# Second MoE of a fused attention and MoE kernel: no row gather in the last unit, no split of weight chunks for an expert that does not exist

## The chip, the cores and the metric

The kernel runs on one core of one Trainium2 chip. The metric is the device time of one execution in microseconds, here the median of three runs. Times "at 422.2" are microseconds from the start of the profiled span.

## What is computed

Three stages follow one another: attention with a local window and global columns, a soft MoE (every slot sees every token), and a top-1 MoE. The change lies wholly in the third, which is this (cut):

```python
logits = x @ w_gate                      # x (3072, 512), 8 experts
expert_idx = np.argmax(logits, axis=1)
gate_w = softmax(logits)[arange(N), expert_idx]
for e in range(E):
    mask = expert_idx == e
    if not mask.any():
        continue
    h = np.maximum(x[mask] @ w1[e], 0.0)
    out[mask] = gate_w[mask, None] * (h @ w2[e])
```

Only the experts that got tokens are computed; how many these are is known at run time alone. The kernel calls that number `used`, and an expert's place in the order of work its `rank`.

## The kernel before, in words

The attention output is stage one's, and x, the input of the third stage, is a product of the 32-slot combine weights with slot outputs. The third stage therefore gathers rows of combine weights (`c_rows` in HBM, 128 floats for a token) and not rows of x. Tokens are sorted by expert into tiles of 128, two tiles are a unit, and the units of all ranks are numbered through (`u`).

One unit goes so. GpSimd gathers the unit's two tiles of rows into `Cg` with two indirect DMAs (`gather`, L1486, each with its index taken from `src1`, which a small copy at L1480 fills). TensorE transposes them (`turn`, L1546), ScalarE copies the transposed rows to `CgT` (L1716), TensorE multiplies them into the folded first weights (`hidden`, L1557), ScalarE takes the ReLU into `hh` (L1724), VectorE makes the low part `hl` (L1913), and TensorE multiplies with the expert's second weights, high and low part, three products for each of eight chunks of the hidden width (`tile`, L1626 to L1628). VectorE scales the tile by its gate (L1986), and GpSimd stores it with an indirect DMA to the token's row of the output (L1513, index in `dst1`, filled at L1509). The work is pipelined by one unit: while TensorE does the products of unit u it also does `turn(u + 1)` and `hidden(u + 1)`, and GpSimd issues the gather for unit u + 2 before the stores of unit u. After the last unit `hidden` still runs once, for a unit that is not there, on whatever was gathered.

The second weights of rank r lie in slot `r & 1` of `w2h` (high part) and `w2l` (low part). Those of ranks 0 and 1 are split in place. Those of rank r + 2 are loaded to `raw` and split in four chunks when rank r is done: ScalarE copies a chunk to `w2h` (L1788, in `rank_done`), VectorE subtracts it from `raw` into `w2l` (L2011). The number of chunks at the end of a rank comes from `chunks_at_end`: four if rank r + 2 exists, else one.

The order of the work is the order in which each engine's code is written, in loops over ranks and units whose bounds are loaded from SBUF at run time (`count`, L1395; `plan`, L1387; `all_units`, L1399). The engines meet by semaphores. At the end of the program every engine runs a DRAIN and then a barrier; the records of both stand under L129. Before that GpSimd waits until all stores have landed (`stored`), reads the number of units (L1399), and waits for all gathers.

Of the kernel before, what the change touches and what calls it, by code (L numbers as in the profile page):

```python
# [15 lines left out]
F32 = mybir.dt.float32  # L16
# [3 lines left out]
ALU = mybir.AluOpType  # L20
# [39 lines left out]
W2CH = 4  # L60
# [1163 lines left out]
def top1_moe(nc, ctx, sb, psum, sem, block, sp_passed, ident, ones, Rsel, wg_sb, mem, STR, CT, counting,  # L1224
# [23 lines left out]
    w2h = sb(st, "w2h", [P, 2, WSIZE], F32R)  # L1248
    w2l = sb(st, "w2l", [P, 2, WSIZE], F32R)
# [19 lines left out]
    act = sb(st, "act", [P, NE])  # L1269
# [34 lines left out]
    raw = mem[:, 0, :]  # L1304
# [38 lines left out]
    v2_loaded = [sem("v2_loaded_first"), sem("v2_loaded_second")]  # L1343
# [3 lines left out]
    w2_high = sem("w2_high")  # L1347
    w2_low = sem("w2_low")
    src_copied = sem("src_copied")
    dst_copied = sem("dst_copied")  # L1350
    gathered = sem("gathered")
# [5 lines left out]
    y_quarter = sem("y_quarter")  # L1357
# [6 lines left out]
    act_passed = sem("act_passed")  # L1364
    dve_passed = sem("dve_passed")
# [3 lines left out]
    def column(t):  # L1369

        return t if isinstance(t, int) else t.with_bounds(min_val=0, max_val=MAXT - 2)
# [13 lines left out]
    def plan(eng, r):  # L1385

        word = eng.value_load(rt[0:1, 1, bass.ds(rank_at(r), 1)], min_val=0, max_val=(1 << 19) - 1)  # L1387
        return ((word & 15).with_bounds(min_val=1, max_val=TT // 2),
                ((word >> 4) & 31).with_bounds(min_val=0, max_val=MAXU - 3),
                ((word >> 9) & 31).with_bounds(min_val=1, max_val=TT),  # L1390
                (word >> 14).with_bounds(min_val=0, max_val=TT + NE - 2))

    def count(eng):

        return eng.value_load(rt[0:1, 2, 0:1], min_val=1, max_val=NE)  # L1395

    def all_units(eng):

        return eng.value_load(rt[0:1, 2, 1:2], min_val=1, max_val=MAXU - 2)  # L1399

    def all_tiles(eng):

        return eng.value_load(rt[0:1, 2, 2:3], min_val=1, max_val=TT + NE - 1)

    def chunks_at_end(rank, used):


        return 1 + (rank + 2 < used) * (W2CH - 1)

    def chunk(ch):  # L1410

        return slice(ch * CW, (ch + 1) * CW) if isinstance(ch, int) else bass.ds(ch * CW, CW)
# [18 lines left out]
    @block.sync  # L1431
    def _(sp):
        sp.wait_ge(experts_known, 1)
        for r in range(2):
            e = number(sp, r)
            if r:

                sp.wait_ge(gathered, 32)
                load_rows(sp, e0, slice(FC // 2, 3 * FC // 4), v2_third)
                load_rows(sp, e0, slice(3 * FC // 4, FC), v2_loaded[0])  # L1440
            else:
                e0 = e
            load_v1(sp, e, r)
            if r:
                load_v2(sp, e, w2l[:, r, :].bitcast(F32), v2_loaded[r])
            else:
                load_rows(sp, e, slice(0, FC // 2), v2_half)
        used = count(sp)
        with sp.If(used > 2):
            with sp.Fori(2, used) as r:  # L1450
                e = number(sp, r)

                sp.wait_ge(gp_done, r * 2)
                sp.sem_inc(sp_passed, 1)
                load_v1(sp, e, 1)
            with sp.Fori(2, used) as r:
                e = number(sp, r)

                sp.wait_ge(w2_low, r * W2CH)
                sp.sem_inc(sp_passed, 1)  # L1460
                load_v2(sp, e, raw, v2_loaded[1])

    @block.gpsimd
    def _(pool):
        pool.sem_inc(y_quarter, 4)
        pool.sem_inc(y_scaled, 2)
        pool.wait_ge(c_stored, 16)
        pool.wait_ge(first_ready, 1)

        def gather(u, turned):  # L1470


            if not isinstance(u, int) or u >= 1:
                pool.wait_ge(gathered, u * 32)
                pool.sem_inc(pool_step, 1)
            if isinstance(u, int):
                index = src_i[:, 2 * u:2 * u + 2] if u else src_0[:]
            else:
                index = src1[:]
                nc.gpsimd.tensor_copy(src1[:], src_i[:, bass.ds(column(u * 2), 2)]).then_inc(src_copied, 1)  # L1480
                pool.wait_ge(src_copied, u - 1)
            if not isinstance(u, int) or u >= 1:
                pool.wait_ge(cg_turned, turned)
            pool.sem_inc(pool_step, 1)
            for i in range(2):
                nc.gpsimd.indirect_dma_start(out=Cg[:, i, :], out_offset=None, in_=c_dram,  # L1486
                                             in_offset=bass.IndirectOffsetOnAxis(ap=index[:, i:i + 1], axis=0)
                                             ).then_inc(gathered, 16)

        gather(0, 0)  # L1490
        pool.wait_ge(v2_half, 16)
        nc.gpsimd.tensor_copy(w2h[:, 0, chunk(0)], w2l[:, 0, chunk(0)].bitcast(F32)).then_inc(w2_first, 1)
        pool.wait_ge(src_ready, 1)
        gather(1, 1)
        pool.wait_ge(rt_ready, 1)
        pool.wait_ge(dst_ready, 1)
        used, total = count(pool), all_tiles(pool)
        with pool.Fori(0, used) as rank:
            units, first, tiles, tile0 = plan(pool, rank)
            with pool.Fori(0, units) as j:  # L1500
                u = first + j
                gather(u + 2, u + 2)

                with pool.Fori(0, 1 + (tiles > j * 2 + 1)) as i:
                    done = tile0 + j * 2 + i

                    pool.wait_ge(row_free, u * 2 + i + 1)
                    pool.sem_inc(pool_step, 1)
                    nc.gpsimd.tensor_copy(dst1[:], dst_i[:, bass.ds(column(u * 2 + i), 1)]).then_inc(dst_copied, 1)  # L1509
                    pool.wait_ge(dst_copied, done + 1)  # L1510
                    pool.wait_ge(y_scaled, u * 2 + i + 3)
                    pool.sem_inc(pool_step, 1)
                    nc.gpsimd.indirect_dma_start(  # L1513
                        out=out_d, out_offset=bass.IndirectOffsetOnAxis(ap=dst1[:, 0:1], axis=0),
                        in_=Ysb, in_offset=None, bounds_check=TOK - 1, oob_is_err=False
                    ).then_inc(stored, 16)

        pool.wait_ge(stored, total * 16)
        pool.sem_inc(pool_step, 1)
        units = all_units(pool)  # L1520
        pool.wait_ge(gathered, (units + 2) * 32)
        pool.sem_inc(pool_step, 1)

    @block.tensor
# [164 lines left out]
    def _(act):  # L1689
# [3 lines left out]
        used = count(act)  # L1693
# [86 lines left out]

        def rank_done(rank, last):

            act.wait_ge(v2_loaded[1], (rank + 1) * (rank + 2 < used) * 16 + 16)
            act.sem_inc(act_passed, 1)
            act.wait_ge(y_quarter, last * 4 + 4)
            act.sem_inc(act_passed, 1)
            with act.Fori(0, chunks_at_end(rank, used)) as ch:
                nc.scalar.copy(w2h[:, bass.ds(rank & 1, 1), chunk(ch)].rearrange("p a f -> p (a f)"),  # L1788
                               raw[:, chunk(ch)]).then_inc(w2_high, 1)

        act.wait_ge(v1_loaded[1], 16)
        for ch in range(W2CH):
# [1 line left out]
        with act.Fori(0, used) as rank:  # L1794
            units, first = plan(act, rank)[0:2]

            with act.If(units > (rank < 1) * 1):
                with act.Fori((rank < 1) * 1, units) as j:
                    u = first + j
                    next_unit(u, expert(u + 2))  # L1800
            rank_done(rank, first + units)

    @block.vector
    def _(dve):
        v = nc.vector
# [143 lines left out]
        used = count(dve)  # L1949
# [45 lines left out]
        with dve.Fori(0, used) as rank:  # L1995
            units, first, _, tile0 = plan(dve, rank)

            with dve.If(units > (rank < 1) * 1):
                with dve.Fori((rank < 1) * 1, units) as j:
                    u = first + j  # L2000
                    scaled(u, 0, tile0 + j * 2)
                    for q in range(3):
                        low(u + 1, q)
                    scaled(u, 1, tile0 + j * 2 + 1)
                    low(u + 1, 3)
            with dve.Fori(0, chunks_at_end(rank, used)) as ch:

                all_done = (rank + 1 < used) + (used < 2)
                dve.wait_ge(w2_high, rank * W2CH + W2CH + 2 + ch + all_done * (W2CH - 1))
                dve.sem_inc(dve_passed, 1)  # L2010
                v.tensor_tensor(w2l[:, bass.ds(rank & 1, 1), chunk(ch)].rearrange("p a f -> p (a f)"), raw[:, chunk(ch)],  # L2011
                                w2h[:, bass.ds(rank & 1, 1), chunk(ch)].rearrange("p a f -> p (a f)").bitcast(F32),
                                ALU.subtract).then_inc(w2_low, 1)

    st.close()

# [43 lines left out]
```

## Time and profile before

| | us |
|---|---|
| median of three runs | 440.76 |
| lowest and highest of the three | 440.45, 442.17 |
| time of the profiled execution | 439.07 |
| its span, first to last instruction | 437.4 |
| TensorE busy | 421.4 (96%) |
| VectorE, ScalarE, GpSimd busy | 239.2, 212.2, 210.0 |
| last matmul of the second MoE ends | 433.1 |

How to read it: PE is TensorE, PEld its weight loads, DVE VectorE, ACT ScalarE, POOL GpSimd, SP SyncE; a q behind a name (DVEq) is the engine's sequencer, which reads instructions, waits on semaphores and branches. L1788 is line 1788 of the kernel. A timeline row gives start, duration, engine, line, operation, what is written and read, and in brackets how long the engine had been idle and who released it.

### The profile page before, as it was taken

What the parts mean: (1) busy time and instruction counts of PE and PEld (TensorE: products, weight loads), DVE (VectorE), ACT (ScalarE), POOL (GpSimd) and SP (SyncE); (2) the same over time, 40 slices, a digit from 0 to 9 for tenths busy, and PEclk for the clock granted to TensorE, in tenths of its full rate; (3) what the DMA queues carried; (4) which work ended last, traced back from release to release, by engine and by line L of the source; (5) the groups of instructions that cost most, each with busy time, mean ns of one, the idle gap of its engine ahead of it and who ended that gap; (6) DMA issues with size and microseconds to landing.
All of it is one profiled execution on the core that took longest, in us unless ns stands there. A gap on an engine that the chain in (4) does not pass through costs nothing.

```text
span 437.4 us, 9412 instructions
## 1 busy us (share of the span) xinstructions
PE 421.4 (96%) x3036; PEld 353.6 (81%) x3037; DVE 239.2 (55%) x791; ACT 212.2 (49%) x418; POOL 210.0 (48%) x216
## 2 busy tenths in 40 slices
PE   8999999999999999998797999999999999999996
PEld 7899999999999997743234977688888888888884
DVE  6667777777767775556100679574333323333344
ACT  3887788788888773422010016373333333332244
POOL 5899999999999910010001020234333344443422
PEclk9999999999999999999999999999999999999999
DMA  7866989898977304999995488511111111112111
GB/s 236 278 220 251 402 345 393 343 364 317 393 262 240 106 21 133 391 391 409 397 386 211 140 294 289 217 55 60 60 53 43 60 60 60 60 36 58 55 54 14
DMA packets 29174, 89.21 MB, mean 204 GB/s; under 512 B 3440, under 2 KB 6000, under 8 KB 29136
## 3 DMA queue, kind: packets, MB, share of 16 engines
q1 hardware_dynamic: 25456, 78.47, 48.4%
q0 software_dynamic: 3360, 9.83, 7.2%
q10 hardware_dynamic: 320, 0.42, 0.4%
q8 instruction: 22, 0.36, 0.3%
q14 instruction: 16, 0.13, 0.1%
HBM read 80.85 MB, written 8.13 MB: 203 GB/s over the span
## 4 chain that ended last, share of the span: by engine, by line
PE 85%; DMA 7%; DVE 3%; issue 2%; ACT 1%; POOL 0%; SPq 0%; ACTq 0%; DVEq 0%; POOLq 0%
PE O L445 17%; PE Yq L1626 11%; PE Yq L1627 10%; PE Yq L1628 10%; PE PT L427 9%; PE S L418 5%; PE S L417 5%; DMA ext<-in_moe_w 5%; PE Gp L1557 3%; DMA w2h<-in_moe_w 2%; PE XTp L893 2%; PE Lp L982 2%; PE Cp L1529 2%; PE O L395 2%; PE Up L902 1%
## 5 line engine op out<-in xcount | busy, mean ns | idle before, releaser
L523 ACT ACTIVATE shared<-shared,nm 128x256 f32<-128x256 f32 (+1 forms) x192 | 83.7, 484 | 30.3 <-DVE nm L636 30.1
L445 PE MATMUL O<-V,PTs 128*128 128x65 f32 x704 | 90.1, 269 | 0.0
L636 DVE CUSTOM_DVE_ANT_0 shared<-S,TA 128x256 f32<-128x256 f32 (+1 forms) x192 | 68.7, 396 | 34.4 <-PE S L418 31.7
L445 PEld LDWEIGHTS O<-V,PTs 128*128 128x128 f32 x704 | 86.5, 191 | 1.1 <-issue 1.0
L1626 PE MATMUL Yq<-w2h,hh 128*128 x208 | 83.0, 399 | 0.4 <-issue 0.4
L1627 PE MATMUL Yq<-w2l,hh 128*128 x208 | 81.2, 390 | 0.0
L1628 PE MATMUL Yq<-w2h,hl 128*128 x208 | 81.2, 390 | 0.0
L380 POOL TENSOR_TENSOR kl<-k_raw,kh 128x816 fp32r<-128x816 f32 x30 | 57.9, 1931 | 5.0 <-ACT kh L538 2.9
L1913 DVE SCALAR_TENSOR_TENSOR hl<-Gp,hh 128x512 fp32r<-128x512 f32 x56 | 38.1, 688 | 39.4 <-ACT hh L1724 39.4
L376 POOL TENSOR_TENSOR qs<-q_raw,qs 64x768 fp32r<-64x768 f32 x30 | 54.7, 1825 | 2.4
L427 PE MATMUL PT<-ident,shared 128*128 128x128 f32 x352 | 54.7, 274 | 0.0
L417 PE MATMUL S<-kh,qs 128*128 128x256 f32 (+1 forms) x180 | 53.0, 317 | 0.0
L1724 ACT ACTIVATE hh<-Gp 128x512 fp32r<-128x512 f32 x56 | 32.9, 600 | 30.4 <-PE Yq L1628 27.4
L1986 DVE TENSOR_SCALAR mem<-Yq,gate_s 128x512 f32<-128x512 f32 x26 | 19.5, 751 | 49.7 <-PE Yq L1628 47.0
L1626 PEld LDWEIGHTS Yq<-w2h,hh 128*128 128x128 f32 x208 | 39.1, 188 | 9.2 <-issue 1.5
L418 PE MATMUL S<-kl,qs 128*128 128x256 f32 (+1 forms) x180 | 46.2, 280 | 0.0
L1628 PEld LDWEIGHTS Yq<-w2h,hl 128*128 128x128 f32 x208 | 39.0, 188 | 8.3
L1627 PEld LDWEIGHTS Yq<-w2l,hh 128*128 128x128 f32 x208 | 39.2, 188 | 7.4 <-issue 0.2
L1486 POOL DMA_INDIRECT Cg<-c_rows,src x28 | 27.6, 986 | 35.2 <-DVE src L1892 19.6
L1513 POOL DMA_INDIRECT out<-mem,dst x25 | 25.5, 1019 | 37.4 <-DVE mem L1986 34.4
L1736 ACT CAST Gst<-mem 128x512 fp32r x28 | 16.0, 617 | 54.7 <-PE Gp L1557 53.3
L427 PEld LDWEIGHTS PT<-ident,shared 128*128 128x128 f32 x352 | 42.1, 156 | 0.3 <-ACT shared L523 0.3
(248 smaller groups left out, 571.7 us busy)
## 6 DMA issues: line engine op xcount, KB each, us to landing
mem<-in_moe_w SPq DMA_DIRECT2D x9, 2048.0 KB, 11.6
ext<-in_moe_w SPq DMA_DIRECT2D x6, 2048.0 KB, 19.8
V<-in_v SPq DMA_DIRECT2D x16, 715.0 KB, 6.8
k_raw<-in_k SPq DMA_DIRECT2D x13, 816.0 KB, 7.0
q_raw<-in_q SPq DMA_DIRECT2D x13, 768.0 KB, 4.6
xmem<-in_moe_w SPq DMA_DIRECT2D x2, 2048.0 KB, 11.1
w2h<-in_moe_w SPq DMA_DIRECT2D x1, 2048.0 KB, 10.2
w2l<-in_moe_w SPq DMA_DIRECT2D x1, 2048.0 KB, 15.5
```

The lines of the kernel that those rows point to most:

```text
L376: nc.gpsimd.tensor_tensor(qs[HD:P, buf, :, cq], q_raw[HD:P, buf, :, cq], qs[HD:P, buf, :, cq].bitcast(F32), ALU.subtract).then_inc(q_split, 1)
L380: nc.gpsimd.tensor_tensor(kl[:, buf, :, ck], k_raw[:, buf, :, ck], kh[:, buf, :, ck].bitcast(F32), ALU.subtract).then_inc(k_split, 1)
L417: pe.matmul(S[par][h][:, 0:w], q, kh[:, buf, h, at:at + w], start=True, stop=False)
L418: mm = pe.matmul(S[par][h][:, 0:w], q, kl[:, buf, h, at:at + w], start=False, stop=True)
L427: mm = pe.transpose(PT[par][:, (h * kbs + kb) * P:(h * kbs + kb + 1) * P], Pb[:, par, h, kb * P:(kb + 1) * P], ident[:])
L445: mm = pe.matmul(O[grp % 2][:, at:at + VC], PTs[:, par, (h * kbs + kb) * P:(h * kbs + kb + 1) * P], V[:, buf, h, vb, :], start=(n == 0), s ...
L523: nc.scalar.activation(Pb[:, par, h, 0:width(g)], Pb[:, par, h, 0:width(g)], ACT.Exp, bias=nm[:, par, h:h + 1], scale=-1.0).then_inc(exp_d ...
L636: v.tensor_tensor_reduce(Pb[:, par, h, 0:w], S[par][h][:, 0:w], tab, -SCALE, HUGE, ALU.add, ALU.min, nm[:, par, h:h + 1]).then_inc(biased, 1)
L1626: pe.matmul(Yq[i][:], h, high[:, cols], start=(fc == 0), stop=False)
L1627: pe.matmul(Yq[i][:], h, low[:, cols], start=False, stop=False)
L1628: mm = pe.matmul(Yq[i][:], rest, high[:, cols], start=False, stop=(fc == FC - 1))
L1913: v.scalar_tensor_tensor(hl[:, q, :], Gp[:, q, :], 0.0, hh[:, q, :].bitcast(F32), ALU.max, ALU.subtract).then_inc(hid_low, 1)
```

## The change

GpSimd's gather at the head of a unit stands behind a condition: it is issued only if another unit follows. The number of units, which was read after the loops, is read before them, once, and the last wait counts one gathered unit less. `chunks_at_end` goes; ScalarE's and VectorE's work at the end of a rank stands behind a condition (rank + 2 < used), and the four chunks in it are written out and not looped over.

```diff
-    def chunks_at_end(rank, used):
-        return 1 + (rank + 2 < used) * (W2CH - 1)
...
-        used, total = count(pool), all_tiles(pool)
+        used, total, last = count(pool), all_tiles(pool), all_units(pool)
         with pool.Fori(0, used) as rank:
             units, first, tiles, tile0 = plan(pool, rank)
             with pool.Fori(0, units) as j:
                 u = first + j
-                gather(u + 2, u + 2)
+
+                with pool.If(u + 1 < last):
+                    gather(u + 2, u + 2)
...
         pool.wait_ge(stored, total * 16)
         pool.sem_inc(pool_step, 1)
-        units = all_units(pool)
-        pool.wait_ge(gathered, (units + 2) * 32)
+
+        pool.wait_ge(gathered, (last + 1) * 32)
         pool.sem_inc(pool_step, 1)
...
         def rank_done(rank, last):
-            act.wait_ge(v2_loaded[1], (rank + 1) * (rank + 2 < used) * 16 + 16)
-            act.sem_inc(act_passed, 1)
-            act.wait_ge(y_quarter, last * 4 + 4)
-            act.sem_inc(act_passed, 1)
-            with act.Fori(0, chunks_at_end(rank, used)) as ch:
-                nc.scalar.copy(w2h[:, bass.ds(rank & 1, 1), chunk(ch)].rearrange("p a f -> p (a f)"),
-                               raw[:, chunk(ch)]).then_inc(w2_high, 1)
+
+            with act.If(rank + 2 < used):
+                act.wait_ge(v2_loaded[1], rank * 16 + 32)
+                act.sem_inc(act_passed, 1)
+                act.wait_ge(y_quarter, last * 4 + 4)
+                act.sem_inc(act_passed, 1)
+                for ch in range(W2CH):
+                    nc.scalar.copy(w2h[:, bass.ds(rank & 1, 1), chunk(ch)].rearrange("p a f -> p (a f)"),
+                                   raw[:, chunk(ch)]).then_inc(w2_high, 1)
...
-            with dve.Fori(0, chunks_at_end(rank, used)) as ch:
-
-                all_done = (rank + 1 < used) + (used < 2)
-                dve.wait_ge(w2_high, rank * W2CH + W2CH + 2 + ch + all_done * (W2CH - 1))
-                dve.sem_inc(dve_passed, 1)
-                v.tensor_tensor(w2l[:, bass.ds(rank & 1, 1), chunk(ch)].rearrange("p a f -> p (a f)"), raw[:, chunk(ch)],
-                                w2h[:, bass.ds(rank & 1, 1), chunk(ch)].rearrange("p a f -> p (a f)").bitcast(F32),
-                                ALU.subtract).then_inc(w2_low, 1)
+            with dve.If(rank + 2 < used):
+                for ch in range(W2CH):
+                    dve.wait_ge(w2_high, rank * W2CH + (2 * W2CH + ch + 1))
+                    dve.sem_inc(dve_passed, 1)
+                    v.tensor_tensor(w2l[:, bass.ds(rank & 1, 1), chunk(ch)].rearrange("p a f -> p (a f)"),
+                                    raw[:, chunk(ch)],
+                                    w2h[:, bass.ds(rank & 1, 1), chunk(ch)].rearrange("p a f -> p (a f)").bitcast(F32),
+                                    ALU.subtract).then_inc(w2_low, 1)
```

GpSimd's code from the head of its loop over units to the end of the program, before (ISA is an arithmetic step on registers; waits and semaphore steps have no rows; `src` is `src1`):

```order
L1500 ISA
L1474 REGISTER_ALU
L1474 ISA
L1480 ISA
L1480 COPY src<-src_i 128x2
L1481 REGISTER_ALU
L1486 DMA Cg<-c_rows,src 128x128 x2
...
L1518 REGISTER_ALU
L1399 TENSOR_LOAD rt
L1399 ISA x2
L1521 ISA
L129 UNCONDITIONAL_BRANCH
```

and with the change:

```order
L1495 UNCONDITIONAL_BRANCH
L1495 ISA
L1498 REGISTER_ALU
L1498 ISA
L1498 COMPARE_AND_BRANCH
L1469 ISA
L1475 ISA
L1475 COPY src<-src_i 128x2
L1481 DMA Cg<-c_rows,src 128x128 x2
...
L1515 REGISTER_ALU
L1518 ISA
L129 UNCONDITIONAL_BRANCH
```

The copy and the two gathers stand behind a compare and branch, and the load of the unit count with its two register steps has gone from between the last two waits (to the place ahead of the loop over ranks, where L1399 now stands behind L1403).

VectorE's code from the end of its loop over units to the end of the program, before:

```order
L1999 COMPARE_AND_BRANCH
L1998 UNCONDITIONAL_BRANCH
L2006 UNCONDITIONAL_BRANCH
L2006 ISA
L2009 ISA
L2011 ISA
L2011 REGISTER_ALU
L2011 ISA
L2011 TENSOR_TENSOR w2l<-mem,w2h 128x1024
L2006 ISA
L2006 COMPARE_AND_BRANCH
```

and with the change:

```order
L1998 COMPARE_AND_BRANCH
L1997 UNCONDITIONAL_BRANCH
L2005 REGISTER_ALU
L2005 COMPARE_AND_BRANCH
...
L2009 TENSOR_TENSOR w2l<-mem,w2h 128x1024
L2007 REGISTER_ALU
L2009 ISA
L2009 TENSOR_TENSOR w2l<-mem,w2h 128x1024
...
L2005 UNCONDITIONAL_BRANCH
```

One subtraction in a loop that always ran at least once has become four, which a branch can pass over. ScalarE's copies (L1788 before, L1787 now) have moved in the same way. TensorE's and SyncE's instructions are the same.

## Rows read from the trace of the kernel before

**Rows 1.** Page, part 1: engine, busy us (share of the span) xinstructions.

```profile
PE 421.4 (96%) x3036; PEld 353.6 (81%) x3037; DVE 239.2 (55%) x791; ACT 212.2 (49%) x418; POOL 210.0 (48%) x216
```

**Rows 2.** Windows of the second MoE: stretch, length, busy us (count) of PE, PEld, DVE, ACT, POOL, clock.

```profile
396.00:420.00 24.00, 24.00 (x117) 20.09 (x116) 8.35 (x12) 7.59 (x15) 9.15 (x14) 1.00 0.21 55
...
433.10:437.40 4.30, 0.00 (x0) 0.00 (x0) 2.63 (x4) 1.64 (x2) 0.00 (x0) 1.00 0.00 0
```

**Rows 3.** Counts by line, ns min/median/max, first and last start: stores, gathers, chunk copies.

```profile
L1513 POOL DMA_INDIRECT out<-mem,dst x25: 998/1024/1082, 287.1 to 429.4; - x25
...
L1486 POOL DMA_INDIRECT Cg<-c_rows,src x28: 945/972/1133, 259.4 to 427.2; - x28
...
L1788 ACT CAST w2h<-mem x2: 1044/1046/1048, 422.2 to 434.3; - x2
```

**Rows 4.** Chain of waits at the end, start, us, what.

```profile
432.87 0.24 PE Yq L1628
...
434.31 1.05 ACT w2h L1788
```

**Rows 5.** Timeline of DVE, 420 to 437.4.

```profile
421.24 0.75 DVE L1986 TENSOR_SCALAR mem<-Yq,gate_s 128x512 f32<-128x512 f32 x1 [0.19 <-PE Yq L1628]
...
423.78 1.23 DVE L2011 TENSOR_TENSOR w2l<-mem,w2h  x1 [1.19 <-ACT w2h L1788]
426.94 0.75 DVE L1986 TENSOR_SCALAR mem<-Yq,gate_s 128x512 f32<-128x512 f32 x1 [1.94 <-PE Yq L1628]
...
434.02 0.68 DVE L1913 SCALAR_TENSOR_TENSOR hl<-Gp,hh 128x512 fp32r<-128x512 f32 x1
435.87 1.22 DVE L2011 TENSOR_TENSOR w2l<-mem,w2h  x1 [1.17 <-ACT w2h L1788]
```

**Rows 6.** Records of the program's end under L129: duration in ns, start.

```profile
L129 POOLq DRAIN  x1: 4655/4655/4655, 432.5 to 432.5; - x1
...
L129 DVEq DRAIN  x1: 791/791/791, 436.4 to 436.4; - x1
...
L129 POOLq EVENT_SEMAPHORE  x2: 17/17/17, 437.2 to 437.3; - x2
```

**Rows 7.** Timeline of POOL in the last units.

```profile
411.80 0.20 POOL L1480 COPY src<-src_i 128x2 int32 x1
...
414.15 0.97 POOL L1486 DMA_INDIRECT Cg<-c_rows,src  x1 [0.30 <-issue]
...
422.91 1.00 POOL L1513 DMA_INDIRECT out<-mem,dst  x1 [1.89 <-DVE mem L1986]
424.72 0.33 POOL L1480 COPY src<-src_i 128x2 int32 x1 [0.81 <-issue]
...
428.17 0.20 POOL L1509 COPY dst<-dst_i 128x1 int32 x1
429.37 1.03 POOL L1513 DMA_INDIRECT out<-mem,dst  x1 [0.99 <-POOL dst L1509]
```

**Rows 8.** POOL's sequencer behind the wait for the stores.

```profile
L1399 POOLq TENSOR_LOAD <-rt x1: 296/296/296, 431.7 to 431.7; - x1
L1399 POOLq FUSED_REGOPS  x1: 153/153/153, 432.1 to 432.1; - x1
```

**Rows 9.** Timeline of ACT at the change of rank.

```profile
410.50 0.37 ACT L1716 CAST CgT<-Cp 128x256 fp32r<-128x256 f32 x1 [0.92 <-PE Cp L1546]
...
422.21 1.05 ACT L1788 CAST w2h<-mem  x1 [0.53 <-issue]
424.32 0.38 ACT L1716 CAST CgT<-Cp 128x256 fp32r<-128x256 f32 x1 [1.06 <-issue]
```

**Rows 10.** Timeline of PE: the turned rows and the products that read them.

```profile
422.19 0.38 PE L1546 MATMUL Cp<-ident,Cg 128*128 128x128 f32 x2
...
426.52 1.11 PE L1557 MATMUL Gp<-CgT,Gst 128*128 128x256 f32 x8
```

**Rows 11.** Chain of waits, an idle time of PE that no record explains.

```profile
166.51 2.75 issue
```

## The prediction

> **What bounds the kernel now.** I read the engines' busy times first: TensorE is busy for 96% of the span [rows 1]. The windows come next. In the stretch of the second MoE shown, TensorE is busy for the whole 24.00 us, at a granted clock of 1.00; in the last 4.3 us it does nothing [rows 2]. So this change has two places in which it can act: on something TensorE waits for, of which there is nothing, or in the tail behind the last matmul at 433.1. The counts show what this input makes of the loops: 28 gathers on L1486 (two more stand on another form of that line), 25 stores, and chunk copies on L1788 only twice, at 422.2 and 434.3 [rows 3]. Thirteen units and two ends of a rank, so `used` is 2: no rank r + 2 ever exists, and both chunk splits of this run are of the kind that the change drops.
>
> The chain of waits shows the tail: last matmul to 433.11, then ReLU and sequencer steps on ScalarE, the chunk copy 434.31 to 435.36, and the chunk subtraction on VectorE, 435.87 to 437.09 [rows 4, 5]. The span ends 0.3 later. Nobody reads that chunk. VectorE's last useful operation ends at 434.70 [rows 5].
>
> The chain names one engine, but the end is a barrier over all, so I read the records of the program's end. VectorE's DRAIN ends with its subtraction, at 436.4 + 0.79 = 437.2. GpSimd's DRAIN starts at 432.5 and lasts 4.66, to 437.15, and its next record is at 437.2 [rows 6]. Two engines thus finish together, within what rounded starts can tell. Taking 2.4 us off VectorE is worth 2.4 only if GpSimd is done as early.
>
> **Why GpSimd's DRAIN ends there.** Either it takes 4.66 us whatever else happens, or VectorE's subtraction holds it up. One row speaks for the second. The small index copy on GpSimd takes 0.20 us in an ordinary unit, but 0.33 at 424.72, where it ends at 425.05; the other chunk subtraction ran from 423.78 to 425.01 [rows 5, 7]. So a GpSimd step that meets this subtraction ends 0.04 behind it, and the DRAIN (437.15 against 437.09) looks alike. The Trainium skill (SBUF — State Buffer, section "SBUF: two separate sides") says that a VectorE operation with two SBUF inputs and a GpSimd operation that reads SBUF exclude each other for a whole instruction; by that rule the DRAIN's own length would be shorter than 4.66, and the trace agrees in the copy's 0.33 against 0.20. If the DRAIN was held, it still had work left when the subtraction began at 435.87, else it would have ended before. Its own length X is then between 435.87 − 432.5 = 3.4 and 437.09 − 432.5 = 4.6; unheld, it is 4.66. No row splits these. I take the middle, X = 4.0, since nothing in the trace is nearer to either end, and keep 3.4 and 4.66 for the range.
>
> **Part 1: no gather in the last unit.** It takes away an index copy, two gathers (0.97 to 1.13 us each) and a wait for TensorE's transposes, all queued ahead of the store of the last real tile. Before: the tile was scaled by 426.94 + 0.75 = 427.69, the store's index copy waited its turn until 428.17, and the store was issued at 429.37 [rows 5, 7]. Where the index is ready in time, the store follows the scaling by 0.92 (421.24 + 0.75 = 421.99, then 422.91) [rows 5, 7]. So it will be issued at 428.61, 0.76 earlier, and land as much earlier. The gathers' own DMAs collide with nothing that is waited for.
>
> **Part 2: the unit count is read ahead of the loops.** Behind the wait for the stores stood a load of 0.30 and register steps of 0.15 [rows 8], with the gaps about 0.5 of the 0.8 between 431.7 and the DRAIN. They go. The DRAIN then starts at 432.5 − 0.76 − 0.5 = 431.2 and ends at 431.2 + 4.0 = 435.2. The same load, paid ahead of the loops, and a register step and a compare and branch in each of thirteen units (below 0.2 us together, as sequencer steps here are 0.03 to 0.15) fall on an engine that TensorE does not wait for: in an ordinary unit the second gather is issued at 414.15 [rows 7]. The last store's wait passes at 431.7, 2.3 after its issue; a gather that takes as long is there at 416.5, and its rows are turned at 422.19 [rows 7, 8, 10], 5.7 later. Cost nothing; if that cover were gone, 0.5 once and 0.2 a unit.
>
> **Part 3: no chunk at the end of rank 0.** Removed are a copy of 1.05 at 422.21 and a subtraction of 1.23 at 423.78 [rows 5, 9]. The copy made `CgT` late: it was written at 424.32 to 424.70, and the products that read it start at 426.52 [rows 9, 10]. It had 1.8 us to spare, so an earlier `CgT` moves nothing. VectorE's next operation waits for TensorE at 426.94. Gain: nothing.
>
> **Part 4: no chunk at the end of rank 1.** The copy and the subtraction go from the tail. VectorE ends at 434.70, its DRAIN at about 434.75, ScalarE ends before it, with its ReLU. That takes 2.4 off this path. The branch passes over four written-out chunks: a register step and a compare and branch that the sequencer does while the last operation runs. Cost nothing.
>
> **Sum.** The tail ends with the later of VectorE (434.75) and GpSimd (435.2), against 437.15: a gain of 1.95, all of it in the tail. The profiled execution would go from 439.07 to 437.1, its span from 437.4 to 435.4. It stands 1.7 below the median of the runs, as one execution with its own offset, so I take the gain from the median: 440.76 − 1.95 = **438.8 us**. With X = 4.66 the DRAIN ends at 435.9 and the gain is 1.25 (439.5); with X below 3.55 VectorE sets the end and the gain is 2.4 (438.4).
>
> About 0.5%, 2.2 us, is what a measurement of this kernel can tell from no change. The forecast lies just inside it.
>
> **The rivals.**
> - **VectorE sets the end.** GpSimd's own DRAIN needs at most 3.75 us, and the gain is 2.2 to 2.4: 438.4. For it: the chain of waits, which names VectorE alone, and the held copy. Against: the subtraction covered 1.2 us of possible ends, and only the first 0.35 of them give this. Chance 0.29.
> - **The DRAIN is tied to something else.** Its end may hang on the last DMA that GpSimd issued, by more than its own wait shows: then it moves with the store alone, by 0.76, or less. Time 440.0. Against it: the stores have landed (the wait has passed) when it starts. Chance 0.09. That the change does not do what it says I count here too; with `used` = 2 the conditions are false in both ranks, so I see no way for it.
> - **Slower: GpSimd's loop has to load its code again in each unit.** GpSimd's loop body grows by some six instructions. If it came to lie across two blocks of code that do not stay loaded, each unit would pay for loads. A wait of TensorE for which no record stands, 2.75 us at 166.51 [rows 11], is the nearest price. Two loads a unit (5.5) fit in the 5.7 us that a gather has to spare; three (8.25) do not, and the 2.55 over it in eleven units would be +28, less the tail's 2: 467. It decides from 5.7 us a unit. Against: TensorE is busy throughout the units of before [rows 2], and the code only grows by a few instructions of a short loop. The Trainium skill (Advanced Engine Details and Errata, "ISA Cache") gives two cache lines of 256 instructions for an engine, by which a loop as short as this stays loaded even across a boundary; no row here shows a line's size. Chance 0.02.
>
> **Chances and range.** The forecast, the DRAIN of GpSimd last with X from 3.75 to 4.66, has 0.60 (438.6 to 439.5). The first rival is beyond 0.5% by a little or nothing, and the forecast's near edge can fall over it: faster 0.34, same 0.64, slower 0.02. The fastest run of before lies 0.3 below the median, and both medians can be off by that: low end 438.4 − 0.6 = 437.8. High end: the DRAIN tied to the store, 440.0, plus 0.3: 440.3.
>
> **What will show it.** L1788's and L2011's successors are absent from the trace; the gathers on their line number 26; the store of the last tile is issued 0.9 behind its scaling; VectorE's last operation still ends 1.6 behind the last matmul. The decisive record is GpSimd's DRAIN: it should start at 431.2, if the last matmul still ends at 433.1, and its length, now that nothing holds it, is X. A length of 4.66 says that it was never held; below 3.6, VectorE's DRAIN is the last. The forecast is wrong if TensorE's busy stretch up to 433.1 changes, or if the DRAIN ends where VectorE's ends again.

## The result

The changed kernel takes 437.60 us (median of 5 executions, 437.21 to 438.48), the kernel before on the same chip 440.45 us (5 executions, 440.07 to 442.17): ratio 0.9932, 95% interval 0.9909 to 0.9955. It is faster; the time is 1.2 us below the forecast and 0.2 us outside the range. Three of the five executions of the kernel before are those behind the 440.76 that the forecast started from.

The profiled execution says something smaller: 437.52 against 439.07, and a span of 435.8 against 437.4, 1.6 us less. The medians lie 2.9 us apart, the two profiled spans only 1.6; both numbers need an account.

The windows of the changed kernel, columns as in [rows 2], show TensorE's work as it was:

```profile
396.00:420.00 24.00, 24.00 (x117) 20.09 (x116) 8.35 (x12) 7.57 (x15) 9.12 (x14) 1.00 0.22 55
```

The end of its chain of waits (start, us, what):

```profile
432.88 0.24 PE Yq L1625
...
434.04 0.67 DVE hl L1912
```

The last matmul ends at 433.12, against 433.11 [rows 4], and VectorE's last operation at 434.71; the copy and the subtraction are gone. All of the gain thus lies behind the last matmul: 4.3 us of tail have become 2.7. Now the records of the program's end, which answer to [rows 6] (duration in ns, start):

```profile
L129 POOLq EVENT_SEMAPHORE  x2: 17/17/17, 435.6 to 435.7; - x2
...
L129 POOLq DRAIN  x1: 4492/4492/4492, 431.1 to 431.1; - x1
...
L129 DVEq DRAIN  x1: 326/326/326, 434.4 to 434.4; - x1
```

VectorE is done at 434.7. GpSimd's DRAIN runs from 431.1 to 435.6, and the barrier closes behind it. The chain of waits names VectorE as the last here too, since it follows operations and a DRAIN is none: the record of the DRAIN has to be looked up. GpSimd's own timeline answers to [rows 7]:

```profile
422.91 1.00 POOL L1510 DMA_INDIRECT out<-mem,dst  x1 [1.89 <-DVE mem L1985]
426.00 0.18 POOL L1506 COPY dst<-dst_i 128x1 int32 x1 [2.09 <-DVEq L1981]
428.58 0.98 POOL L1510 DMA_INDIRECT out<-mem,dst  x1 [2.40 <-DVE mem L1985]
```

The gathers of the last unit are gone (26 records on their line, 28 before), the index copy for the store is done long before it is needed, and the store is issued at 428.58, 0.79 earlier.

### The profile page after: what moved, and what is told of

It reads as the page before. It is cut to its first block, busy times and chain, and to the rows that moved or that the text cites. A ratio compares the mean times of both kernels' runs of the same rounds, so it can differ in the third digit from the quotient of the medians.

```text
span 435.8 us, 9380 instructions
## 1 busy us (share of the span) xinstructions
PE 420.6 (97%) x3036; PEld 352.3 (81%) x3037; DVE 236.8 (54%) x789; ACT 209.9 (48%) x416; POOL 207.5 (48%) x213
## 4 chain that ended last, share of the span: by engine, by line
PE 69%; POOL 11%; DMA 9%; DVE 5%; issue 4%; ACT 2%; SPq 0%; POOLq 0%; DVEq 0%; ACTq 0%
PE Yq L1623 11%; PE Yq L1624 11%; PE Yq L1625 11%; PE O L445 9%; POOL kl L380 5%; PE PT L427 5%; POOL qs L376 5%; DMA ext<-in_moe_w 5%; PE Gp L1554 3%; PE S L418 3%; PE S L417 3%; DMA k_raw<-in_k 2%; PE XTp L893 2%; PE Lp L982 2%; DMA mem<-in_moe_w 2%
## 5 line engine op out<-in xcount | busy, mean ns | idle before, releaser
L1481 POOL DMA_INDIRECT Cg<-c_rows,src x26 | 25.7, 987 | 33.9 <-DVE src L1891 19.7
```

## The experiments

**Each part alone.** The first four kernels had three questions: does each part work alone, does the 2.9 us between the medians come back, and where does an execution of the kernel before that takes longer lose its time? The edits: none (`before_again`, `after_again`), the diff of GpSimd's block alone (`pool_only`), the diff of `rank_done` and of VectorE's last lines alone (`chunks_only`).

> The kernel before, unchanged, as a kernel of its own. Theory A (the change shortens the tail by 1.6 us, and the rest of the 2.9 us between the medians is a difference between executions that has nothing to do with the change): this kernel's executions spread over 438 to 442, its profiled span lies anywhere between 437.2 and 439.5, and where it is above 437.4 the extra sits ahead of the second MoE (in the attention or the soft MoE), while the last matmul ends 4.3 us before the end of the span, as before. Theory B (the tail of the kernel before is longer in ordinary executions than in the one profiled): a profiled span above 437.4 shows its extra behind the last matmul.

> The change to GpSimd's code alone; ScalarE and VectorE still split one chunk at the end of each rank. Theory A (the end is the later of VectorE's last operation and GpSimd's DRAIN, which takes 4.49 us by itself): the DRAIN starts near 431.2 and ends near 435.7, but VectorE's subtraction still ends at 437.1, so the span gains 0.0 to 0.1 us over the kernel before. Rival (GpSimd's DRAIN alone sets the end, VectorE's work is beside it): gain 1.6 us in the span.

> The change to ScalarE's and VectorE's code alone; GpSimd still gathers in the last unit and reads the unit count after the stores. Theory A (the later of the two): VectorE is done at 434.75, GpSimd's DRAIN starts at 432.5 and takes its own 4.49 us to 436.97, so the span gains 0.15 us. If VectorE's subtraction held the DRAIN up, its length is 4.49 here against 4.66 before. Rival (VectorE's path alone sets the end): gain 1.6 to 2.4 us.

> The changed kernel once more, on the same chip as the three others. Both theories: the last matmul ends near 433.1 and the span 2.7 us later; GpSimd's DRAIN takes 4.49 us. Theory A: the ratio to the kernel before varies from session to session around 0.9965, with the executions' spread; Theory B: it stays at 0.993.

Measured, 12 executions each against 35 of the kernel before (median 440.07): before_again 439.82, ratio 1.0010 [0.9987, 1.0033]; pool_only 440.24, 1.0009 [0.9991, 1.0027]; chunks_only 440.03, 1.0004 [0.9989, 1.0018]; after_again 438.20, 0.9972 [0.9955, 0.9988]. **Neither part alone moves the time, both together do.** In the records under L129, of pool_only:

```profile
L129 POOLq DRAIN  x1: 4492/4492/4492, 431.7 to 431.7; - x1
...
L129 DVEq DRAIN  x1: 793/793/793, 437.0 to 437.0; - x1
```

and of chunks_only:

```profile
L129 POOLq DRAIN  x1: 4655/4655/4655, 432.8 to 432.8; - x1
...
L129 DVEq DRAIN  x1: 322/322/322, 434.9 to 434.9; - x1
```

Without GpSimd's gathers the DRAIN is over at 436.2, but VectorE's subtraction ends at 437.8. Without the subtraction VectorE is over at 435.2, but the DRAIN ends at 437.5. Each time the other engine holds the span, as Theory A said: the span ends 4.2 us behind the last matmul in pool_only and 4.1 in chunks_only, against 4.3 before, where it forecast gains of 0.0 to 0.1 and 0.15. One expectation fell at once: in chunks_only no subtraction is there to hold the DRAIN up, and it takes 4.655 us, to the nanosecond the length of before. Its length goes with the gathers and not with VectorE. That it had ended within 0.1 us of the subtraction in the kernel before was chance.

chunks_only also answers for the index copy that had pointed to a hold. The same copy, 0.81 us behind the store as before, but with no subtraction beside it:

```profile
425.23 0.19 POOL L1475 COPY src<-src_i 128x2 int32 x1 [0.81 <-issue]
```

With the subtraction it takes 0.33 us in both profiles of the kernel before, without it 0.19. So the subtraction does hold this copy, and does not hold the DRAIN.

On the spread: before_again's profiled span is 437.6, its last matmul ends 4.3 us before the end of it, as in the first profile, and the 0.2 us more lie ahead of that matmul. Its twelve executions run from 438.69 to 444.17 us, one of them beyond the 442 that was expected; the 35 others of the kernel before run from 438.61 to 441.77. Over the twelve executions of after_again the spans run from 435.5 to 438.4, and the three of 438.1 and more all have a mean granted clock of 0.988, while those at 1.000 lie between 435.7 and 436.5. The windows show where the clock was lower. Columns as in [rows 2], first the kernel before, then before_again, of the stretch 217 to 225 in the soft MoE:

```profile
217.00:225.00 8.00, 7.66 (x68) 2.81 (x68) 0.02 (x1) 1.17 (x2) 0.00 (x0) 1.00 1.05 386
```

```profile
217.00:225.00 8.00, 8.00 (x64) 2.17 (x56) 0.00 (x0) 0.59 (x1) 0.00 (x0) 0.84 1.05 386
```

So executions of one kernel differ by 3 us and once by 5.5, and at least part of that goes with TensorE's clock far ahead of the change. Executions with the same mean clock can be compared with each other. These are medians of the span, in us, of the 47 executions of the kernel before (before_again and the 35) and the 12 of after_again, with the number of executions:

| mean granted clock | kernel before | changed kernel | difference |
|---|---|---|---|
| 1.000 | 437.6 (4) | 436.0 (4) | 1.6 |
| 0.996 | 437.4 (10) | 436.4 (4) | 1.0 |
| 0.988 | 439.8 (8) | 438.15 (4) | 1.65 |

At equal clock the difference is 1.0 to 1.65 us, and two of the three rows give the 1.6 of the tail. That is a ratio of 0.9964: inside the interval of after_again and just outside that of the first five executions. As for the remaining 1.2 us of their 2.9, all five of the changed kernel ran at 0.996 to 1.000. The clocks of the five of the kernel before are not known. Their median, 440.45, would be a span of about 438.75 (an estimate: in these executions the time is 1.65 to 1.8 us above the span). The 69 other executions of the kernel before have a median span of 437.8 at a clock of 0.995 or more, and of 438.8 below it. So it is likely that the five ran at the lower clocks and that this made most of the 1.2 us; it is not shown.

**What sets the DRAIN's length.** The kernel before issues 56 DMAs from GpSimd (30 gathers, 25 stores, one of `c_rows`), the changed one 54. 4.655 and 4.492 differ by 0.163, or 0.0815 a DMA, and 4.492 is 54 times 0.083. To tell a count over the whole program from what is recent, eight small loads were added early, in the changed kernel (`extra8`) and in pool_only (`pool_extra8`), which also moves the DRAIN's end into VectorE's subtraction:

```diff
+        for i in range(8):
+            nc.gpsimd.dma_start(extra[:, i, :], v2_d[0, 0:P, i * 16:(i + 1) * 16]).then_inc(extra_in, 16)
         pool.wait_ge(src_ready, 1)
+        pool.wait_ge(extra_in, 8 * 16)
```

> The changed kernel with 8 small DMAs more on GpSimd's queue, issued at about 263 to 271 us in an idle time of GpSimd and waited for at once; their data is read by nobody. Theory C (GpSimd's DRAIN takes 0.083 us for each DMA that GpSimd issued in the whole program: 4.655 us for 56, 4.492 us for 54): the DRAIN takes 62 x 0.0832 = 5.16 us and the span ends 0.67 us later. Rival D (its length comes from the gathers of the last unit or from what is recent): it stays at 4.49 us.

> The same 8 DMAs in the kernel that has only GpSimd's part of the change, where VectorE's chunk subtraction (two operands in SBUF) still runs 2.8 to 4.0 us behind the last matmul. The DRAIN, if it takes 5.16 us, would end 3.3 us behind the last matmul, in the midst of the subtraction. Theory C without a hold: length 5.16. The theory of my prediction (the subtraction holds GpSimd's DRAIN until it is over): the DRAIN ends 0.04 us behind the subtraction and is about 0.7 us longer than in extra8, 5.8 to 5.9 us.

Records of extra8 under L129:

```profile
L129 POOLq DRAIN  x1: 5140/5140/5140, 432.9 to 432.9; - x1
```

and of pool_extra8, with VectorE's subtraction from its timeline:

```profile
L129 POOLq DRAIN  x1: 5140/5140/5140, 432.2 to 432.2; - x1
```

```profile
436.98 1.23 DVE L2018 TENSOR_TENSOR w2l<-mem,w2h  x1 [1.17 <-ACT w2h L1795]
```

5.140 us both times, 0.648 more for 8 DMAs, 0.081 each, although they were issued and waited for 160 us earlier. Their size does not matter: one of these loads moves 8 KB, a gather 64 KB, and both cost 0.081 to 0.082 us. In pool_extra8 the DRAIN ends at 437.3, in the midst of the subtraction (436.98 to 438.21), and is not a nanosecond longer. The subtraction does not hold the DRAIN. Each was executed once (439.94 and 440.19 us), too few to compare the times.

**No DRAIN, and a DRAIN in each unit.** `no_drain` is the changed kernel with one edit; `unit_drain` has a DRAIN behind the unit's stores:

```diff
-        block = nc.Block()
+        block = nc.Block(no_gpsimd_drain=True)
```

```diff
                     ).then_inc(stored, 16)
+                with pool.If(u + 1 < last):
+                    pool.drain()
```

> The changed kernel, with a block end in which GpSimd runs no DRAIN (all its DMAs are waited for before). Theory C and Theory A both: the end is then VectorE's last operation, 1.6 us behind the last matmul, and the span ends some 0.3 later, 1.9 to 2.0 us behind the last matmul and not 2.7; 0.8 us faster than the changed kernel, ratio to the kernel before 0.9953. Rival: another engine or the barrier takes the DRAIN's place and nothing is gained.

> The changed kernel, with a DRAIN on GpSimd at the end of each unit but the last. Theory C, with the DRAIN clearing what it has counted: the last DRAIN has one store in it and takes 0.1 to 0.4 us; each one inside takes a wait for the store to land and 0.3 us, in time that GpSimd has; the span ends as without the DRAIN, 0.8 us earlier than the changed kernel. Rival E (a DRAIN always walks over all DMAs of the program, or costs a fixed few us): the last one still takes 4.5 us, and each inside one takes up to that; a gather then comes late for TensorE and the kernel is several us slower.

no_drain: 438.09 (7 executions), ratio 0.9946 [0.9926, 0.9965]. In its profile the last matmul ends at 432.64 and the span at 434.6, 2.0 later and not 2.7: VectorE's end, 434.23, now sets it, as expected. The medians alone would not have told this from the changed kernel; the tail in the profile does.

unit_drain: 453.0 us, ratio 1.0286 [1.0255, 1.0318]. Here the expectation failed, in its second half:

```profile
L129 POOLq DRAIN  x1: 137/137/137, 450.7 to 450.7; - x1
```

The last DRAIN takes 0.137 us, so a DRAIN does clear the count. But each of the twelve inside took 2.70 to 3.05 us, right behind a store that has still to land, and GpSimd comes late to the next gather and store. A unit takes 13.4 us and not 12.1. The waits show who paid (in total us, times, longest), over 282 to 452:

```profile
DVE mem L1987 <- DMA out<-mem,dst: 85.8, 24, 4.0
...
PEld Yq L1625 <- DVE hl L1914: 13.7, 11, 1.5
```

VectorE waits for the first tile's store before it may overwrite `Ysb`, its low parts come late, and TensorE's weight loads wait 13.7 us for them, eleven times. In the changed kernel the two waits are 5.8 and 0.4 us.

**The DRAIN in an idle time, and the wasted work of the last unit.** GpSimd is idle for 3.3 us between the first tile's store and the second tile's index copy. `i_drain` puts the DRAIN there. `tail_cut` leaves the DRAIN at the end and takes work away: the last unit no longer transposes, multiplies, takes a ReLU or makes low parts for a unit that is not there, and does not compute its second tile, which holds no tokens with these inputs.

```diff
                     done = tile0 + j * 2 + i
+                    with pool.If(i > 0):
+                        pool.drain()
```

```diff
-            tile(u, 0, rank, high, low)
-            hidden(u + 1)
-            tile(u, 1, rank, high, low)
+            tile(u, 0, rank, high, low, ahead=u + 1 < last)
+            with pe.If(u + 1 < last):
+                hidden(u + 1)
+            with pe.If((u + 1 < last) + full > 0):
+                tile(u, 1, rank, high, low)
```

(`ahead` guards the transposes; `full` is `tiles > j * 2 + 1`; ScalarE and VectorE have the same conditions, and GpSimd leaves out the gather of one unit more, so that it issues 52 DMAs.)

> The changed kernel, with a DRAIN on GpSimd in each unit between the first tile's store and the wait for the second tile's turn, where GpSimd stands idle for 3.3 us. Theory C (0.081 us for each DMA since the last DRAIN, and a wait until they have landed): each inner DRAIN ends before GpSimd is asked for the next index copy, the units keep their 12.11 us, the last DRAIN has two stores in it and takes 0.2 to 0.3 us, and the span ends 1.9 to 2.0 us behind the last matmul, as without a DRAIN: 0.8 us under the changed kernel, ratio to the kernel before about 0.994. Rival (a DRAIN in a unit always delays the loop): units longer than 12.11 us and a slower kernel, as with a DRAIN at the unit's end.

> The changed kernel, and besides the last unit does nothing for a unit behind it (no transposes, no products into the hidden layer, no ReLU, no low parts), and its second tile, which holds no tokens here, is not computed. TensorE's work ends with the first tile's products, about 6 us earlier. Theory C (the end is: first tile scaled, stored, landed, DRAIN of 0.081 x 52 + 0.12 = 4.33 us): the store comes at most 0.3 us earlier (the transposes), the DRAIN is 0.16 us shorter (two gathers fewer), so the span gains only 0.4 to 0.5 us over the changed kernel although 6 us of TensorE's work is gone. Rival (the work behind the last store still sets the end): gain of 2 us and more.

> The last two together. Theory C: the last DRAIN takes 0.2 to 0.3 us from the landing of the last store at about 430.8 on, so the span ends at about 431.5, 4.3 us under the changed kernel and 5.9 under the kernel before: ratio 0.9866.

> The shortened last unit with no DRAIN on GpSimd at all. Theory C: as with the DRAIN in each unit or 0.2 to 0.4 us less, a span of 431.2: ratio to the kernel before 0.986. Rival: the branches and conditions cost TensorE time in each unit, and units are longer than 12.11 us.

i_drain: 437.66 (6 executions), ratio 0.9947 [0.9931, 0.9963]. Its second index copies, 12.11 us apart as before, and its last DRAIN:

```profile
409.96 0.18 POOL L1508 COPY dst<-dst_i 128x1 int32 x1 [3.31 <-DVEq L1983]
...
422.07 0.18 POOL L1508 COPY dst<-dst_i 128x1 int32 x1 [3.31 <-DVEq L1983]
```

```profile
L129 POOLq DRAIN  x1: 218/218/218, 432.3 to 432.3; - x1
```

The twelve inner DRAINs take 2.57 to 2.77 us each and do not make a unit longer, since they lie in GpSimd's wait. The last of them, with the store ahead of it:

```profile
L1504 POOLq DRAIN  x1: 2569/2569/2569, 418.1 to 418.1; - x1
```

```profile
417.73 1.03 POOL L1512 DMA_INDIRECT out<-mem,dst  x1 [1.07 <-DVE mem L1987]
```

It ends at 420.7, 1.4 us before the wait does and 2.9 behind the issue of the store. In the changed kernel the wait for the last store passes 2.5 us after its issue (428.58, 431.1). With the 0.38 us that four DMAs would cost by then, that makes 2.9 as well (an estimate): the inner DRAIN fits a wait for the store to land, and the DRAIN's own cost behind it. The span ends 1.9 us behind the last matmul (434.34, 436.2) and not 2.7; against after_again the ratios alone would not show it.

tail_cut: 437.67 (7 executions), ratio 0.9952 [0.9937, 0.9968]. TensorE stops 8.95 us before the end of the span instead of 2.7, and next to nothing is won against the changed kernel. Its store of the last tile, and the DRAIN:

```profile
428.40 0.75 DVE L1991 TENSOR_SCALAR mem<-Yq,gate_s 128x512 f32<-128x512 f32 x1 [3.87 <-PE Yq L1625]
```

```profile
430.05 0.99 POOL L1510 DMA_INDIRECT out<-mem,dst  x1 [1.95 <-DVE mem L1991]
```

```profile
L129 POOLq DRAIN  x1: 4328/4328/4328, 432.5 to 432.5; - x1
```

52 DMAs, 4.328 us. In the changed kernel the scaling of the same tile is this:

```profile
426.94 0.75 DVE L1985 TENSOR_SCALAR mem<-Yq,gate_s 128x512 f32<-128x512 f32 x1 [4.35 <-PE Yq L1625]
```

From its start to the end of the span are 8.86 us (426.94 to 435.8) in the changed kernel and 8.70 (428.40 to 437.1) in tail_cut: 0.16 less, as much as the DRAIN is shorter, though the ends are rounded to 0.1. The gain in the median over after_again is 0.5, as expected, with intervals that overlap. The reading stands: 6 us of TensorE's work were hidden behind a store and a DRAIN.

Both edits together, tail_cut_drained: 434.20 (4 executions), ratio 0.9865 [0.9839, 0.9891]; expected 0.9866. The four spans are 431.9 to 433.9, all above the 431.5 expected; from the scaling of the last real tile to the end of the span the profile has 4.65 us (429.25 to 433.9) in place of 8.86, 4.2 less, where 4.3 was expected. Shortened with no DRAIN, tail_cut_no_drain: 434.18 (4), 0.9872 [0.9846, 0.9897]. The medians can't tell the two apart; from the same scaling the profile has 4.3 us (427.77 to 432.1). Its units still take 12.11 us (second index copies at 398.20, 410.31 and 422.43), so the branches cost TensorE nothing. The DRAIN at the end of the first:

```profile
L129 POOLq DRAIN  x1: 216/216/216, 433.4 to 433.4; - x1
```

**These two beat both kernels**, by some 5.8 us against the kernel before and 4 against the changed one (which was measured on another chip). The one with the DRAIN in each unit keeps the DRAIN at the program's end, at the price of 0.3 us.

## The DRAIN in one table

| kernel | GpSimd's DMAs since the last DRAIN | DRAIN, us | 0.055 + 0.082 N |
|---|---|---|---|
| unit_drain, last | 1 | 0.137 | 0.137 |
| i_drain / tail_cut_drained, last | 2 | 0.218 / 0.216 | 0.219 |
| tail_cut | 52 | 4.328 | 4.319 |
| after, after_again, pool_only | 54 | 4.492 | 4.483 |
| before, before_again, chunks_only | 56 | 4.655 | 4.647 |
| extra8, pool_extra8 | 62 | 5.140 | 5.139 |

The line of the last column was drawn through the rows of N = 1 and 62; the others lie within 0.01 us. It is a fit to these kernels, whose gathers, stores and added loads are all of 128 rows; whether a DMA of fewer rows costs less was not tried. It holds where every DMA has already landed.

## Why the prediction was right and where it failed

- **What bounds the kernel, and that both parts can act in the tail alone: right.** The last matmul ends at 433.12; parts 1 and 3 changed nothing ahead of it. At the end of rank 0 `CgT` is written at 423.37 and not 424.32, and nobody noticed.
- **The end is the later of VectorE and GpSimd: right,** and shown by the parts alone, which give nothing each.
- **Part 1 and part 2: right.** The store was forecast at 428.61 (428.58), the DRAIN's start at 431.2 (431.1).
- **X, the DRAIN's own length: the term that was mis-sized.** I read the ends at 437.15 and 437.09, and the index copy of 0.33 us, as a hold by VectorE's subtraction, and put X in the middle between 3.4 and 4.6. It is 4.655 for 56 DMAs and 4.492 for 54, held by nothing (chunks_only, pool_extra8). The term was 4.0 and measured 4.49, so the gain in the span was 1.6 and not 1.95. The end that I had kept for the range, unheld 4.66, was nearly right. This error made the forecast too fast, while the time came out faster still: it is not what put it outside the range. The index copy is held, 0.33 us against 0.19 in chunks_only; this agrees with the exclusive lock of the Trainium skill (SBUF — State Buffer, section "SBUF: two separate sides"). What no row had shown was the step from the copy to the DRAIN.
- **The first rival, VectorE sets the end,** is false for the changed kernel; it became true in no_drain and i_drain, where the DRAIN is out of the way. The second rival (DRAIN tied to the store alone) is false: it started 1.4 us earlier, 0.79 of it from the store. The third (GpSimd's loop loads its code again in each unit) is false: the units still take 12.11 us, and TensorE is as busy in them as before.
- **From the span to the median: the step that put the number outside the range.** I took the gain from a median of three executions and allowed 0.6 for both medians. Executions of one kernel spread by 3 us and more, and the medians of the kernel before were 440.76, 440.45, 440.07, 440.45 and 439.95. The two first medians lie 1.25 us further apart than the spans of the two profiles. At equal mean clock the difference is 1.0 to 1.65 us, so what was added came from the executions, most of it likely from TensorE's clock ahead of the change, and not from the change. Against 440.07 and with 1.6 us of gain the forecast would be 438.5; after_again measured 438.20. That 1.95 lies near the 1.87 between those two medians is luck: the tail gives 1.6. The forecast of a difference within 0.5% was wrong by the first five executions (0.68%) and right by the next twelve (0.28%).

## What to carry to other kernels

The end of a program is a barrier over all engines: list when each one's last record ends before costing a tail, the DRAINs among them, which the chain of waits does not name. If two ends lie within tenths of each other, an edit to one is worth next to nothing, and both together are worth the distance to the later of the two new ends, or to a third engine's. Where GpSimd issues many DMAs, give it a DRAIN in an idle time inside the loop that covers it (here 3.3 us for a DRAIN of up to 2.8), and only then cut the compute behind the last store. Before a difference between two medians is put down to a change, compare executions at equal clock.

## What the runs showed of the hardware that I had not expected

- GpSimd's DRAIN takes 0.055 + 0.082 us for each DMA that GpSimd issued since the last DRAIN, even if that landed 160 us ago: 0.137 us for 1, 5.140 us for 62. Different programs with equal counts agree to the nanosecond (4.492 three times, 4.655 three times).
- A DRAIN clears that count (0.137 us for the last one of unit_drain). Right behind a store it takes 2.57 to 3.05 us, which fits a wait for the store to land.
- A VectorE subtraction with two operands in SBUF, under way while the DRAIN ended, did not lengthen it (5.140 us with and without, 4.655 with and without). It did lengthen a small index copy on GpSimd (0.33 us with, 0.19 without).
